# Moving the token-block sums from GpSimd to VectorE, two units at a time, and the factors s and b to the ends of the last layer

## The reference, cut to what matters

```python
x = moe(attention(q, k, v))            # 4608 tokens x 512
h = x @ w_in                           # 4608 x 2048, w_in is 512 x 2048
r = np.maximum(h, 0.0)
g = s * (r * r) + b                    # s, b: one number each
return (g @ w_out).astype(np.float32)  # w_out is 2048 x 512
```

## Time and profile before

| | us |
|---|---|
| median of the runs | 702.1 |
| lowest and highest run | 702.01, 702.57 |
| the profiled execution, its own time | 698.97 |
| its span from first to last instruction | 697.2 |
| first PE unit of the easy stage starts | 251.2 |
| first `high` and last `high` of the hard stage start | 317.2, 688.3 |

### The profile page before, as it was taken

One profiled execution on the slowest core, in us unless ns is written; L12 is line 12 of the kernel. 1 busy time (PEld: TensorE's weight loads), 2 busy tenths in 40 slices (PEclk: granted clock), 3 DMA queues, 4 the chain that ended last, 5 costly groups with the idle time before them and its releaser, 6 DMA issues.

```text
span 697.2 us, 17047 instructions
## 1 busy us (share of the span) xinstructions
PE 649.5 (93%) x6450; PEld 549.8 (79%) x6450; DVE 489.5 (70%) x710; ACT 437.0 (63%) x735; POOL 511.9 (73%) x537
## 2 busy tenths in 40 slices
PE   7788999999998887588999999999999999999997
PEld 6566677777633355467999999999999999999997
DVE  5757585656136478796777777777777777777775
ACT  1577777876302263576777776777677767777773
POOL 3898776623010057848999999999999999999994
PEclk9899999999998999999999999999999999999999
DMA  9688969582599900001000000000000000000001
GB/s 336 215 260 328 330 244 351 194 339 101 181 362 432 388 1 1 1 0 62 1 31 16 31 16 30 15 23 22 30 15 15 30 30 15 15 30 30 16 17 61
DMA packets 25237, 80.50 MB, mean 115 GB/s; under 512 B 6496, under 2 KB 14688, under 8 KB 22368
## 3 DMA queue, kind: packets, MB, share of 16 engines
q1 hardware_dynamic: 25184, 79.76, 30.8%
HBM read 70.32 MB, written 9.44 MB: 114 GB/s over the span
## 4 chain that ended last, share of the span: by engine, by line
POOL 44%; PE 27%; issue 12%; DVE 9%; ACT 3%; DMA 3%; POOLq 1%; DVEq 0%; ACTq 0%
POOL a_sb L799 17%; POOL a_sb L803 16%; POOL a_sb L805 9%; PE bank L1538 4%; PE bank L1462 2%; PE bank L1621 2%; DVE a_sb L1264 2%; PE bank L1525 2%; PE bank L1495 2%; DVE lo_sb L1270 2%; DMA kvbuf<-in_k_dram 2%; PE bank L1642 2%; PE bank L1568 1%; PE bank L1584 1%; PE bank L1421 1%
## 5 line engine op out<-in xcount | busy, mean ns | idle before, releaser
L1276 DVE TENSOR_TENSOR lo_sb<-a_sb,hi_sb 128x896 fp32r<-128x896 f32 x128 | 141.2, 1103 | 89.5 <-ACT hi_sb L1002 86.3
L1002 ACT ACTIVATE hi_sb<-a_sb 128x896 fp32r<-128x896 f32 x128 | 122.1, 954 | 110.8 <-POOL a_sb L805 109.5
L1264 DVE SCALAR_TENSOR_TENSOR a_sb<-r_sb,sb_col 128x512 f32<-128x512 f32 x144 | 140.0, 972 | 11.4 <-ACT r_sb L980 11.3
L805 POOL TENSOR_TENSOR a_sb<-a_sb 128x128 f32<-128x128 f32 x128 | 125.9, 984 | 10.0
L799 POOL TENSOR_TENSOR a_sb<-a_sb 128x256 f32<-128x256 f32 x128 | 122.1, 954 | 5.1 <-DVE t_late L1257 4.9
L1749 PE MATMUL bank<-w_hi,hi_sb 128*128 128x256 f32 x384 | 114.5, 298 | 3.7 <-issue 1.0
L803 POOL TENSOR_TENSOR a_sb<-a_sb 128x128 f32<-128x128 f32 x128 | 109.0, 851 | 10.0
L1750 PE MATMUL bank<-w_lo,hi_sb 128*128 128x256 f32 x384 | 108.6, 283 | 0.0
L1751 PE MATMUL bank<-w_hi,lo_sb 128*128 128x256 f32 x384 | 108.5, 283 | 0.0
L980 ACT ACTIVATE r_sb<-bank 128x512 f32<-128x512 f32 x144 | 84.1, 584 | 28.3 <-PE bank L1672 25.6
L986 ACT ACTIVATE a_sb<-a_sb,sb_col 128x512 f32<-128x512 f32 x128 | 91.5, 715 | 0.0
(11 more groups left out here) (173 smaller groups left out, 1409.3 us busy)
## 6 DMA issues: line engine op xcount, KB each, us to landing
early_third<-in_moe_w_dram SPq DMA_DIRECT2D x6, 2048.0 KB, 14.0
kvbuf<-in_k_dram SPq DMA_DIRECT2D x12, 768.0 KB, 5.4
kvbuf<-in_v_dram SPq DMA_DIRECT2D x12, 768.0 KB, 6.4
out_dram<-o_sb SPq DMA_DIRECT2D x36, 256.0 KB, 2.3
qbuf<-in_q_dram SPq DMA_DIRECT2D x8, 1024.0 KB, 8.5
early<-in_moe_w_dram SPq DMA_DIRECT2D x4, 2048.0 KB, 12.3
late<-in_moe_w_dram SPq DMA_DIRECT2D x4, 2048.0 KB, 19.8
win_sb<-in_moe_w_in_dram SPq DMA_DIRECT2D x4, 1024.0 KB, 5.5
```

What stands on the lines that cost most here:

```text
L805: pool.tensor_tensor(a[:, 7 * P:8 * P], a[:, 6 * P:7 * P], a[:, 3 * P:4 * P], ALU.subtract).then_inc(s_made, 1)
L1002: act.activation(hi_sb[:, n % 2, :], a_sb[:, n % ARING, P:2 * CH], ACT.Copy).then_inc(hi_ready, 1)
L1264: dve.scalar_tensor_tensor(out=a_sb[:, n % ARING, 0:CH], in0=r_sb[:, n % 2, :], scalar=sb_col[:, 0:1], in1=r_sb[:, n % 2, :], op0=ALU.mult ...
L1276: dve.tensor_tensor(lo_sb[:, n % 2, :], a_sb[:, n % ARING, P:2 * CH], hi_sb[:, n % 2, :].bitcast(F32), ALU.subtract).then_inc(lo_ready, 1)
```

## The change

In words, for each part:

- `gate` and `add_b` go. ACT squares relu (`square`) right behind `relu`, without s and b. `high_easy` is a plain copy and `low_easy` a plain subtraction.
- `token_sums` goes to DVE and treats two units with one set of three instructions. It stands ahead of `low` in the odd units of a group.
- `combos(2)` to `combos(7)` and all eight `combos_low` go to DVE; POOL keeps `combos(0)` and `combos(1)`.
- s enters where products are read from PSUM: `keep_tile`, `keep_p1` and the joins, which become five instructions (three of 256 columns, two of 512) with a per-partition scalar, placed in units k = 2 to 6.
- b enters as one row added to every output tile: b times the column sums of `w_out`. PE makes the sums with a matrix of ones (`sum_rows`, 16 matmuls of 512 columns after unit 5 of the first group), ACT scales them (`scale_row`), POOL adds the two halves and then adds the row to every tile (`add_row`, 512 columns), except the last tile, which DVE does. A store waits for that addition.

```diff
             def token_sums(n, c, k):
-                a = a_sb[:, n % ARING, :]
-                pool.wait_ge(gate_ready, c * KP + (k + 1))
-                pool.tensor_tensor(a[:, 4 * P:6 * P].rearrange("p (x f) -> p x f", x=2), a[:, P:3 * P].rearrange("p (x f) -> p x f", x=2),
-                                   a[:, 0:P].unsqueeze(1).to_broadcast([P, 2, P]), ALU.subtract).then_inc(s_made, 1)
...
+                x = n % ARING
+                a = a_sb[:, x:x + 2, :]
+                before = (c * (SUMS * KP // 2)) + SUMS * (k // 2)
+                dve.wait_ge(g_ready, step(c, k) + 2)
+                dve.wait_ge(lo_ready, step(c, k) - 2)
+                dve.tensor_tensor(a[:, :, 4 * P:6 * P].rearrange("p n (x f) -> p n x f", x=2),
+                                  a[:, :, P:3 * P].rearrange("p n (x f) -> p n x f", x=2),
+                                  a[:, :, 0:P].unsqueeze(2).to_broadcast([P, 2, 2, P]), ALU.subtract).then_inc(s_made, 1)
+                dve.wait_ge(s_made, before + 1)
+                dve.tensor_tensor(a[:, :, 6 * P:7 * P], a[:, :, P:2 * P], a[:, :, 5 * P:6 * P], ALU.add).then_inc(s_made, 1)
+                dve.wait_ge(s_made, before + 2)
+                dve.tensor_tensor(a[:, :, 7 * P:8 * P], a[:, :, 3 * P:4 * P], a[:, :, 6 * P:7 * P], ALU.subtract).then_inc(s_made, 1)
...
+            def square(n, u, before):
+
+                act.wait_ge(r_ready, u + 1)
+                if before:
+                    act.wait_ge(lo_ready, u - ARING + 1)
+                act.activation(a_sb[:, n % ARING, 0:CH], r_sb[:, n % 2, :], ACT.Square).then_inc(g_ready, 1)
...
+            def add_row(m):
+                pool.tensor_tensor(o_sb[:, m, :], o_sb[:, m, :], row_b, ALU.add).then_inc(out_ready, 1)
+
+            def add_rows(c, odd, final):
+                pool.wait_ge(joined, c * JOINS + 3)
+                add_row(2 * odd)
+                if not final:
+                    pool.wait_ge(joined, c * JOINS + JOINS)
+                    add_row(2 * odd + 1)
...
                 for k in range(KP):
                     n = KP * odd + k
+                    if k % 2 and not (final and k == KP - 1):
+                        if first and k == 1:
+                            dve.wait_ge(t_lo_ready, KP)
+                        token_sums(n + 1, c, k + 1)
                     low(n, step(c, k))
-                    if not (final and k >= KP - 3):
-                        gate(n + 3, step(c, k) + 3, True)
+                    if first and k == 0:
+                        combos_low(KP - 1)
                     if first and k in (0, 1):
                         keep_tile(2 * k + 1)
-                    if not first and k < PARTS7:
-                        join(c - 1, 1 - odd, k)
+                    if not first and 2 <= k < 2 + JOINS:
+                        join(c - 1, 1 - odd, k - 2)
...
+                    if first and k == 5:
+                        sum_rows()
```

More of the change, by code:

```diff
@@ L711, in _ @@
                              w_out[i * half:(i + 1) * half, :].rearrange("(p c) f -> p c f", p=P)).then_inc(wout_in[i], 16)
[L713 to L716, removed]
+            for m in range(MT):
+                sp.wait_ge(out_ready, m + 1)
+                sp.dma_start(tile_rows(m), o_sb[:, m, :]).then_inc(stored[m], 16)
             for c in range(HALVES):
-                for m, last in ((0, 4), (1, 7)):
-                    sp.wait_ge(joined, PARTS7 * c + last)
+                for m in range(2):
+                    if c == HALVES - 1 and m == 1:
+                        sp.wait_ge(out_last, 1)
+                    else:
+                        sp.wait_ge(out_ready, MT + 2 * c + m + 1)
                     sp.dma_start(tile_rows(MT + 2 * c + m), o_sb[:, 2 * (c % 2) + m, :]).then_inc(stored[2 * (c % 2) + m], 16)
@@ L809, in _ @@
                 pool.wait_ge(wout_in[i], 16)
-            for k in range(KP):
+            for k in range(POOL_COMBOS):
                 combos(k)
[L812 to L823, removed]
+            pool.wait_ge(row_scaled, 2)
+            pool.tensor_tensor(row_b[:, 0:LEFT], row_d, row_b[:, LEFT:D], ALU.add).then_inc(row_done, 1)
+            pool.wait_ge(row_done, 1)
+            for m in range(MT):
+                pool.wait_ge((o_act, o_dve)[m % 2], m // 2 + 1)
+                add_row(m)
+            with pool.Fori(0, HALVES - 2, 2) as c:
+                add_rows(c, 0, False)
+                add_rows(c + 1, 1, False)
+            add_rows(HALVES - 2, 0, False)
+            add_rows(HALVES - 1, 1, True)
         @block.scalar
@@ L1025, in steps @@
                         relu(n + 3, step(c, k) + 3, bank[7], True)
-                    if not (final and k >= KP - 2):
-                        add_b(n + 2, step(c, k) + 2)
+                        square(n + 3, step(c, k) + 3, True)
+                    if first and k == 0:
+                        combos_high(KP - 1)
+                    if first and k == KP - 1:
+                        scale_row()
             keep_part(0)
@@ L1286, in after, with scaled_sum, both @@
                     return c * PARTS7 + n
-                left, right = slice(0, LEFT), slice(LEFT, D)
+                def scaled_sum(dst, found, scale, addend):
+                    return dve.scalar_tensor_tensor(out=dst, in0=found, scalar=scale, in1=addend, op0=ALU.mult, op1=ALU.add)
+                def both(at):
+                    return half_pair(odd, at).rearrange("p (x f) -> p x f", x=2)
+                s_col = sb_col[:, 0:1]
                 first, second = 2 * odd, 2 * odd + 1
@@ L1352, in _ @@
             steps(HALVES - 1, 1, False, True)
-            for n in range(PARTS7):
+            for n in range(JOINS):
                 join(HALVES - 1, 1, n)
+            dve.wait_ge(joined, HALVES * JOINS)
+            dve.tensor_tensor(o_sb[:, MT - 1, :], o_sb[:, MT - 1, :], row_b, ALU.add).then_inc(out_last, 1)
         @block.tensor
@@ L1711, in products, with sum_rows @@
                         issued += 1
+            def sum_rows():
+                pe.wait_ge(ones_ready, 1)
+                pe.wait_ge(t_lo_ready, KP)
+                pe.wait_ge(o_dve, 1)
+                for k in range(KP):
+                    for part in range(2):
+                        last = pe.matmul(bank[ACC_B[1]][:, :], ones[:, :], t_of(part, k)[:, LEFT * T3:LEFT * COMBOS],
+                                         start=(k == 0 and part == 0), stop=(k == KP - 1 and part == 1))
+                last.then_inc(row_psum, 1)
             def half_blocks(k):
```

163 lines of the change are left out of this document (87 added, 76 removed).

## The result

The changed kernel took 699.21 us (median of 20 runs, 697.70 to 706.28), the kernel before 703.65 on the same chip (20 runs, 698.96 to 708.67). The ratio is 0.9941, with an interval of 0.9918 to 0.9965: 0.6% faster, some 4 us, where 10.5 were forecast. The profiled execution of the change has a span of 696.4; that of before, one of its fastest, 697.2. What follows compares these two stretch by stretch, so it accounts for 0.8 us. The rest of the 4 us is that the median of before lies 4.7 us above its profiled execution and that of after only 1.0 above its own; where the slower executions of before lose that, no trace here shows.

A forecast was written before the change was run, and what follows sets the result against it. The prediction took PE to be paced by POOL, whose sums ACT and DVE follow. Its terms, -20.7 + 10.4 + 1.1 + 3.65 - 6.0 + 0 + 1.05 = -10.5, took 702.1 to 691.6 us, range 680 to 701.

The forecast's parts named there:

- PE's floor in the hard stage: Hard stage: without POOL's work, units come at PE's own 2.76 us instead of 2.922, saving 20.7 us.
- Row addition: Hard stage, unit 4: POOL's row addition delays DVE's second sum; PE loses 0.69 us in each of 15 groups, +10.4.
- The second collision: Hard stage, unit 6: row addition and sums meet again, but DVE is ahead by then; loss 0 to 0.1 us.
- the row's way: Port sharing read from a profile row: the waiting operation begins before the other's recorded end; loss 0.69 us, not 0.86.
- First four additions: Start of the second hard group: four row additions in one POOL piece, mostly covered by `sum_rows`' lateness, +1.1 us (0 to 3).
- `sum_rows`: First hard group: 16 matmuls of 512 columns with nothing beside them on PE, +3.65 us.
- The end: End of the kernel: chained joins and the last tile's row addition finish later, +1.05 us.
- Easy stage: Easy stage: POOL's blocking of DVE goes, four exposed relu waits stay; waste 12.8 instead of 18.8 us, -6.0.
- Handover: Easy to hard stage: `high` stops waiting, but `combos_high(7)` and DVE's work make unit 1 about 2.3 us late; net 0.
- the first (additions hidden): Hard stage: POOL's row additions slip in beside `low`'s waits or hold the port shorter; 680.2 us, chance 0.17.
- the third (both collisions): Hard stage: row additions cost both times, 1.84 us a group, 27.6 in place of 10.4; 708.8 us, chance 0.12.
- The second: Easy stage: ACT becomes the bound, with no gain there, +6.0 us; 697.6 us, chance 0.16.

The follow-up runs named there:

- the fillers: Nine unread matmuls on PE ahead of each of units 6, 7, 9 and 10 of the easy stage, against the changed kernel: 696.46 us.
- run with relu behind high: Changed kernel with ACT's relu and square of a coming block moved behind `high_easy` in the easy stage: 683.66 us, ratio to before 0.976.
- three edits: Changed kernel with relu and square behind `high_easy`, row additions released later, and the first four released one at a time: 666.48 us, ratio to before 0.9474.
- kernel with the first additions apart: Changed kernel with POOL's first four row additions released one at a time instead of in one piece: 697.83 us, ratio to before 0.9899.

## Why the prediction was off

The direction held, and so did the mechanisms that the prediction named. The size did not, 0.6% where 1.5% was forecast: it gave no price to the lower clock behind the waits that stay. Step by step, by the two traces:

- **PE's floor in the hard stage (-20.7)**: right. `high` waits for PE, and nearly every unit without a collision takes 2.76; with the row additions moved, whole groups take 22.08.
- **Row addition (+10.4)**: right in place and cause, a little small. Unit 4 loses 0.74 (forecast 0.69), unit 5 0.10 and unit 7 0.03 more, 0.87 in all: 13.0 for 15 groups. The second collision does take place (POOL's addition at 501.98 takes 1.68 and DVE's second sum 1.41 again), and the 0 to 0.1 that the prediction gave it was right. By the row's way the loss behind unit 4 is 0.69, by which the second sum starts ahead of POOL's recorded end; it did, in effect at 498.39 - 0.42 = 497.97, 0.14 before POOL's recorded end of 498.11. The rule of the Trainium skill that the prediction cites (page "SBUF — State Buffer", section "Who interferes with whom": a block for the whole instruction) would have given 0.86 there. The measured 0.74 lies nearer the row.
- **First four additions (+1.1)**: mis-sized. They cost 5.42 - 2.76 = 2.66 in group 1's first unit. I had the lateness that `sum_rows` leaves cover most of their 5.8 us. All three sums fell into POOL's piece instead (342.4 to 348.9).
- **`sum_rows` (+3.65)**: 6.40 - 2.76 = 3.64, right.
- **The end (+1.05)**: from the last matmul to the end of the span 4.98 against 3.83, +1.15. The last line of the table is off for another reason: PE's part of group 15 takes 22.4 us in both kernels, so nothing of the 0.7 that the forecast has there was to be won.
- **Easy stage (-6.0)**: this is the step that failed. Its waits were right: "four of about 2.7" came as 2.2 to 2.6, 9.7 in all where 10.8 were forecast. What I allowed for what stands behind them, "0.4 for restarts", was 6.2 us of PE at a lower granted clock, which the fillers took out. The earlier trace rows had shown it, with 0.76 granted behind a single wait of 2.97, and I counted that as waste which the change removes, instead of pricing it for each wait that stays.
- **Handover (0)**: the wait is 5.31 - 2.76 = 2.55 against 2.3 forecast, but behind it the clock fell again. The next two units took 3.92 and 3.19, 1.6 us more:

```profile
320.00:325.00 5.00, 4.71 (x27) 4.71 (x28) 3.35 (x6) 2.26 (x5) 0.00 (x0) 0.68 0.01 3
```

The run with relu behind high and that with three edits had as long a wait there (2.16) and no slow unit behind it, so this part isn't fixed either.

The clock thus cost 6.2 + 1.6 = 7.8 us in places where the prediction had 0.4. That, the 1.6 of the first additions and 2.6 of the row additions (13.0 against 10.4) make 11.6; the earlier first unit gives 3.1 back. The two traces miss the forecast by 10.5 - 0.8 = 9.7, the medians by 10.5 - 4.4 = 6.1. The 1.2 between 8.5 and 9.7 is in small terms: 1.0 in the easy stage, 0.25 in the handover's wait, 0.2 in group 1, 0.5 in the last group, less the 0.9 by which the table's way of counting differs from the prediction's. The Trainium skill, page "TensorE: Matmul & The Clock Gate", section "HAM oscillation — how this bites in real kernels", describes a kernel whose TensorE waits 3 to 5 us for transfers between its bursts, and which starts every burst at the lower clock. The trace agrees in kind, with 0.70, 0.84 and 0.78 in three windows in a row behind shorter waits of 2.2 to 2.6; but not every time, as the pair of waits in the kernel with the first additions apart shows.

Of the rivals, the first (additions hidden) fell with 0.87 lost in every group, the third (both collisions) because the loss stayed well under 1.39. The second came out near the time, 697.6, for a wrong reason: ACT wasn't full, it stood in the wrong order and the clock paid for it.

## What to carry to other kernels

Price each wait of TensorE that stays with what follows it, from a wait of the same length in the trace: here about 1.5 us of slow matmuls behind each wait of 2.2 to 2.6, whenever the clock fell. When work is taken off one engine, look at the order on the engine that is late next: the change is worth some 12 us in the easy stage, and four lines in the wrong order on ACT hid them all. And an addition on POOL that nobody waits for still has a place: started one unit later, it costs nothing, and in the middle of DVE's chain 0.87 us a group.

## What the runs showed of the hardware

- Waits of 2.2 to 2.6 us ahead of two neighbouring units, twice, brought the granted clock down to 0.70 to 0.84 over ten us: matmuls of 512 columns at 0.42 apart (the level of 1.2 GHz) in place of 0.228 (2.4 GHz). It did so behind all four waits in the changed kernel's execution, and behind two of the four in the kernel with the first additions apart, whose code for that stage is the same. Single waits did the same at times: behind the 2.15 us at the handover the clock was 0.68 over five us in the changed kernel and 1.00 in the one with relu behind high. So this cost isn't fixed by the waits alone.
- A POOL addition and a DVE addition that both read two SBUF blocks ran one after the other in both directions: POOL's took 1.68 in place of 1.30 with a DVE sum of 0.68 in its way, and DVE's next 1.41 in place of 0.42.
- Sums of two blocks with a strided or repeated operand took no longer than plain additions of as many columns: 0.68 for 512, 0.42 for 256.
- `square` of 512 columns takes 0.63 on ACT, no more than a copy:

```profile
L997 ACT ACTIVATE a_sb<-r_sb x144: 629/632/637, 244.1 to 678.8; 128x512 f32<-128x512 f32 x144
```
